# Attention on one core: row maxima from a one-pass rough score, and scores computed already turned

## The reference

```python
# attention: q, k, v of (2, 8, 576, 64), s of (2, 8, 576)
scores = q @ k.T / sqrt(64)
cum = cumsum(maximum(s, 0))
bias = -(cum[:, None] - cum[None, :])            # decay
scores = where(causal, -1e9, scores + minimum(bias, 0))
attn = exp(scores - max(scores));  attn /= sum(attn) + 1e-9
x = attn @ v                                     # 1152 tokens of 512
# then a sparse mixture of 8 experts (top 2 of noisy gate logits),
# then a dense mixture of 8 experts whose weights are balanced in 8 Sinkhorn rounds
```

## Time and profile before

| | us |
|---|---|
| median of 3 runs | 1273.04 (1272.57 to 1276.03) |
| the profiled execution's own time | 1273.47 |
| its span, first to last instruction | 1271.7 |
| TensorE busy in the span | 1220.6 (96%) |
| VectorE, ScalarE, GpSimd busy | 504.1, 373.2, 108.9 |

### The profile page before, as it was taken

The page is one execution under the profiler, slowest core; times in us unless marked ns, Lnnn a source line. Parts: engine busy times, 40 slices in busy tenths (PEclk is TensorE's granted clock), DMA queues, the critical chain, the costliest instruction groups (busy, mean ns, idle before and its releaser), DMA issues.

```text
span 1271.7 us, 17649 instructions
## 1 busy us (share of the span) xinstructions
PE 1220.6 (96%) x6721; PEld 1093.6 (86%) x6721; DVE 504.1 (40%) x1140; ACT 373.2 (29%) x678; POOL 108.9 (9%) x83
## 2 busy tenths in 40 slices
PE   5999759999999979999999999999999999999998
PEld 4989658888888868999999999999999999999997
DVE  4666665555555541443233233124214214213311
ACT  3666424444444432122122122122113113112110
POOL 2333110011110441000000000000000000000000
PEclk9999869999999979999999999999999999999999
DMA  9690405455554523011012002001101101100000
GB/s 226 179 244 12 143 26 178 178 178 178 178 178 175 164 80 133 1 66 67 1 55 78 0 7 100 25 0 66 66 0 66 66 0 66 66 0 0 25 25 25
DMA packets 23927, 105.54 MB, mean 83 GB/s; under 512 B 4400, under 2 KB 9008, under 8 KB 19792
## 3 DMA queue, kind: packets, MB, share of 16 engines
q1 hardware_dynamic: 17456, 88.51, 20.6%
q0 software_dynamic: 3360, 11.01, 3.0%
q10 hardware_dynamic: 3072, 5.51, 1.3%
HBM read 94.76 MB, written 10.26 MB: 83 GB/s over the span
## 4 chain that ended last, share of the span: by engine, by line
PE 91%; DMA 3%; DVE 3%; issue 1%; ACT 1%; SPq 1%; POOL 0%; POOLq 0%; DVEq 0%; ACTq 0%
PE bank L597 14%; PE bank L596 14%; PE bank L595 14%; PE bank L577 13%; PE bank L579 13%; PE bank L578 13%; PE bank L517 3%; DMA k_raw<-in_kT 2%; PE bank L498 2%; PE bank L480 1%; PE bank L483 1%; PE bank L541 1%; PE bank L629 1%; DMA x_sb<-x_dram,gather_at 1%; PE bank L482 0%
## 5 line engine op out<-in xcount | busy, mean ns | idle before, releaser
L577 PE MATMUL bank<-xTh,w1h 128*128 128x384 f32 (+1 forms) x1024 | 343.2, 335 | 3.0 <-DVE xTl L997 1.6
L578 PE MATMUL bank<-xTl,w1h 128*128 128x384 f32 (+1 forms) x1024 | 340.8, 333 | 0.0
L579 PE MATMUL bank<-xTh,w1l 128*128 128x384 f32 (+1 forms) x1024 | 340.7, 333 | 0.0
L792 ACT ACTIVATE hh<-bank 128x384 fp32r<-128x384 f32 (+1 forms) x256 | 123.1, 481 | 655.0 <-PE bank L579 655.0
L597 PE MATMUL bank<-w2h,hl 128*128 128x512 f32 (+1 forms) x768 | 302.3, 394 | 0.0
L596 PE MATMUL bank<-w2l,hh 128*128 128x512 f32 (+1 forms) x768 | 300.7, 392 | 0.0
L595 PE MATMUL bank<-w2h,hh 128*128 128x512 f32 (+1 forms) x768 | 299.8, 390 | 0.0
L1017 DVE SCALAR_TENSOR_TENSOR hl<-bank,hh 128x384 fp32r<-128x384 f32 (+1 forms) x256 | 139.5, 545 | 367.4 <-ACT hh L792 367.4
L577 PEld LDWEIGHTS bank<-xTh,w1h 128*128 128x128 f32 x1024 | 193.9, 189 | 5.5 <-issue 2.1
L578 PEld LDWEIGHTS bank<-xTl,w1h 128*128 128x128 f32 x1024 | 194.0, 189 | 1.2
L579 PEld LDWEIGHTS bank<-xTh,w1l 128*128 128x128 f32 x1024 | 193.8, 189 | 0.0
(11 more groups left out here) (169 smaller groups left out, 699.7 us busy)
## 6 DMA issues: line engine op xcount, KB each, us to landing
raw<-in_w SPq DMA_DIRECT2D x16, 2048.0 KB, 8.6
raw<-in_w1b SPq DMA_DIRECT2D x8, 2048.0 KB, 7.7
raw<-in_w2b SPq DMA_DIRECT2D x8, 2048.0 KB, 7.6
q_raw<-in_qT SPq DMA_DIRECT2D x16, 288.0 KB, 5.8
k_raw<-in_kT SPq DMA_DIRECT2D x16, 288.0 KB, 7.3
cumj<-cum_dram SPq DMA_DIRECT2D x8, 576.0 KB, 7.8
y_dram<-x_sb ACTq DMA_DIRECT2D x16, 256.0 KB, 4.1
x_dram<-x_sb SPq DMA_DIRECT2D x1, 2304.0 KB, 9.3
```

The lines of the kernel that those rows point to most:

```text
L577: pe.matmul(dst, w1h[:, c, fs], xTh[:, c, ts], start=(c == 0), stop=False)
L578: pe.matmul(dst, w1h[:, c, fs], xTl[:, c, ts], start=False, stop=False)
L579: mm = pe.matmul(dst, w1l[:, c, fs], xTh[:, c, ts], start=False, stop=(c == DC - 1))
L792: act.activation(hh[:, f, 0:n_cols], bank[:, f % UP_BANKS, 0:n_cols], ACT.Relu).then_inc(st.hh_ready, 1)
```

## The change

- Steps now run through one half after the other (`unit_of(k)` is `k // 5`); within a half the exact scores go through tiles of keys, not of queries.
- A new `rough` matmul, 11 steps ahead on TensorE: high part of q against high part of k, in one pass, with two more contraction rows, in which ones meet the high part and remainder of the cumulative sum. VectorE (`row_max`) adds the causal mask in SBUF and takes the negated maximum of the row into the third column of `aug`.
- TensorE turns those columns (`turn_max`, two groups a half), and ScalarE places them (`place_max`) as rows 64 to 66 of `q_top`, below the high part of q.
- `scores` computes the transposed score of one tile of keys against all later queries: `k_top` (high part of k, two rows of the cumulative sum, one of ones) against `q_top`, then `k_two` (high part over remainder) against `q_two` (remainder over high part). Decay and maximum arrive as contraction rows.
- ScalarE takes the exponential straight from PSUM into `probT`. The transposes of probabilities, their copies and the mask matmul are gone. GpSimd cuts the diagonal tile with an `affine_select` (`cut`), for which `mix` waits.
- q is loaded once and k twice; the second places of the high parts are filled by SBUF to SBUF DMAs on SP's queue (`double_k`, `double_q`). GpSimd takes the remainders in eight pieces of 288 columns a head, between its cuts.
- `k_top` lies in the memory of `w1l`, `k_two` in `w2h`, `q_top` in `w2l`; GpSimd's remainder of `w1` therefore waits for the last exact score.
- At the start three more small VectorE operations split the cumulative sum into two parts, and two rows of it are stored and reloaded.

```diff
--- before
+++ after
...
+        q_top = [w2l_flat[0:AUG, i * N:(i + 1) * N] for i in range(HEADS_RING)]
+        k_top = [w1l_flat[0:AUG, i * N:(i + 1) * N] for i in range(HEADS_RING)]
+        k_two = [w2h_flat[:, i * N:(i + 1) * N] for i in range(HEADS_RING)]
...
+        MAX_BANKS, MAX_AT, SCORES_AT, OUT_AT = 3, 3, 4, 6
+        ROUGH_AHEAD, SCORES_AHEAD = 11, 3
+
+        LOW_CHUNKS = 4
+        LOW_COLS = N // LOW_CHUNKS
+        LOWS = 2 * LOW_CHUNKS
+        K_HIGH_AHEAD, Q_HIGH_AHEAD, LOW_AHEAD = 16, 15, 13
...
+        def turns_at(k):
+
+            first, rest = divmod(k + ROUGH_AHEAD - 3, STEPS), divmod(k + ROUGH_AHEAD - 6, STEPS)
+            found = []
+            if first[1] == 0 and 0 <= first[0] < G:
+                found.append((first[0], 0))
+            if rest[1] == 0 and 0 <= rest[0] < G:
+                found.append((rest[0], 1))
+            return found
+
+        TURNED = ((3, 4), (0, 1, 2))
...
         @block.sync
...
+                w = h % HEADS_RING
+                sp.dma_start(k_top[w][HD:HD + 1, :].bitcast(F32), cum_dram[h:h + 1]).then_inc(cum_loaded[w], 16)
+                sp.dma_start(k_top[w][HD + 1:HD + 2, :].bitcast(F32), low_dram[h:h + 1]).then_inc(cum_loaded[w], 16)
+
+            def double_k(h):
+                w = h % HEADS_RING
+                sp.wait_ge(k_high, h + 1)
+                sp.dma_start(k_top[w][0:HD, :].bitcast(F32), k_two[w][0:HD, :].bitcast(F32)).then_inc(k_doubled[w], 16)
+
+            def double_q(h):
+                sp.wait_ge(q_high, h + 1)
+                sp.dma_start(q_two[HD:P, h % Q_RING, :].bitcast(F32), q_top[h % HEADS_RING][0:HD, :].bitcast(F32)).then_inc(q_doubled[h % Q_RING], 16)
...
+                sp.wait_ge(low, LOWS * (h - 1))
+                load_raw(h)
+                if h >= HEADS_RING:
+                    sp.wait_ge(scores_ready, HEAD * (h - HEADS_RING + 1))
+                    load_cum(h)
                 if h >= V_RING:
-                    sp.wait_ge(mixed, HEAD * (h - V_RING + 1) + RING)
-                load_v(h)
+                    sp.wait_ge(mixed, HEAD * (h - V_RING + 1))
+                    load_v(h)
                 if h == 4:
                     for c, g in enumerate((wg, wn, gate2)):
                         sp.dma_start(gates[:, :, c * E:(c + 1) * E], g).then_inc(gates_loaded, 16)
                     sp.dma_start(raw1[:], w1[0]).then_inc(SP_.raw1_loaded, 16)
                     sp.dma_start(raw2[:], w2[0]).then_inc(SP_.raw2_loaded, 16)
-
-            sp.wait_ge(head_done, G + 4)
+                double_k(h)
+                sp.wait_ge(scores_ready, HEAD * (h - Q_RING + 1))
+                double_q(h)
...
         @block.gpsimd
...
+            def low_part(h, c, k):
+                cols = slice(c % LOW_CHUNKS * LOW_COLS, (c % LOW_CHUNKS + 1) * LOW_COLS)
+                if c < LOW_CHUNKS:
+                    if c == 0:
+                        if h and k <= 0:
+                            pool.wait_ge(low, LOWS * h)
+                        pool.wait_ge(q_high, h + 1)
+                        if h >= Q_RING:
+                            pool.wait_ge(scores_ready, HEAD * (h - Q_RING + 1))
+                    to, raw, high = q_two[0:HD, h % Q_RING, cols], q_raw[:, h % RAW_RING, cols], q_top[h % HEADS_RING][0:HD, cols]
+                else:
+                    if c == LOW_CHUNKS:
+                        pool.wait_ge(k_high, h + 1)
+                    pool.wait_ge(low, LOWS * h + c)
+                    if k > 0:
+                        pool.wait_ge(causal_done, k)
+                    to = high = k_two[h % HEADS_RING][HD:P, cols]
+                    raw = k_raw[HD:P, h % RAW_RING, cols]
+                pool.tensor_tensor(to, raw, high.bitcast(F32), ALU.subtract).then_inc(low, 1)
+
+            def cut(k):
+                h, c = low_at(k)
+                if h is not None and c >= LOW_CHUNKS:
+                    pool.wait_ge(low, LOWS * h + c + 1)
+                n, j = unit_of(k), k % STEPS
+                wide = rows_in(j)
+                pool.wait_ge(prob_ready, k + 1)
+                diag = probT[0:wide, n % UNIT_RING, PROB_AT[j]:PROB_AT[j] + wide]
+                pool.affine_select(out=diag, in_=diag, pattern=[[1, wide]], compare_op=ALU.is_ge,
+                                   fill=0.0, base=0, channel_multiplier=-1).then_inc(causal_done, 1)
+
+            for k in range(-LOW_AHEAD, ALL):
+                h, c = low_at(k)
+                if h is not None:
+                    low_part(h, c, k)
+                if k >= 0:
+                    cut(k)
...
+            pool.wait_ge(scores_ready, ALL)
             for c in range(DC):
...
         @block.tensor
...
+            def rough(k):
+                h, b, t = head_of(k), half_of(k), rough_tile(k)
+                w, rows, width = h % HEADS_RING, rows_in(t), min(S, (t + 1) * P)
                 if k % HEAD == 0:
+                    pe.wait_ge(q_high, h + 1)
+                    if h == 0:
+                        pe.wait_ge(k_first, 1)
+                    else:
+                        pe.wait_ge(k_doubled[w], 16 * (h // HEADS_RING + (w > 0)))
+                    pe.wait_ge(cum_loaded[w], 32 * (h // HEADS_RING) + 32)
+                if k >= 2:
+                    pe.wait_ge(max_ready, k - 1)
+                first = (0, 2, 0, 1, 2)[k % STEPS]
+                q = q_top[w][0:HD + 2, b * S + t * P:b * S + t * P + rows]
                 for c0 in range(0, width, BANK):
                     c1 = min(width, c0 + BANK)
+                    mm = pe.matmul(bank[0:rows, first + c0 // BANK, 0:c1 - c0], q, k_top[w][0:HD + 2, b * S + c0:b * S + c1],
+                                   start=True, stop=True)
+                mm.then_inc(rough_ready, 1)
+
+            def turn_max(n, part):
+                tiles = TURNED[part]
+                pe.wait_ge(max_ready, STEPS * n + (2 if part == 0 else STEPS))
+                if n or part:
+                    pe.wait_ge(max_placed, 2 * n + part)
+                for t in tiles:
+                    rows = rows_in(t)
+                    at = (t - tiles[0]) * P
+                    mm = pe.transpose(bank[0:3, MAX_AT, at:at + rows], aug[0:rows, n % MAX_RING, t, :], ident[0:rows, 0:rows])
+                mm.then_inc(max_turned, 1)
+
+            def scores(k):
+                n, h, b, s_ = unit_of(k), head_of(k), half_of(k), k % STEPS
+                w = h % HEADS_RING
+                if k % HEAD == 0:
+                    pe.wait_ge(low, LOWS * (h + 1))
+                    pe.wait_ge(q_doubled[h % Q_RING], 16 * (h // Q_RING) + 16)
+                if s_ == 0:
+                    pe.wait_ge(max_placed, 2 * n + 2)
+                if k >= 2:
+                    pe.wait_ge(prob_ready, k - 1)
+                pieces = ((s_, s_ * P, S if s_ else ST * P, 0),) if s_ < ST else ((0, ST * P, S, 0), (ST, ST * P, S, HALF))
+                for j, i0, i1, at in pieces:
+                    wide = rows_in(j)
+                    c = slice(b * S + j * P, b * S + j * P + wide)
+                    r_ = slice(b * S + i0, b * S + i1)
+                    dst = bank[0:wide, SCORES_AT + k % 2, at:at + i1 - i0]
+                    pe.matmul(dst, k_top[w][:, c], q_top[w][:, r_], start=True, stop=False)
+                    mm = pe.matmul(dst, k_two[w][:, c], q_two[:, h % Q_RING, r_], start=False, stop=True)
                 mm.then_inc(scores_ready, 1)
...
-            def turn(k):
...
+            for k in range(-ROUGH_AHEAD, ALL):
+                if k + ROUGH_AHEAD < ALL:
+                    rough(k + ROUGH_AHEAD)
+                for n, part in turns_at(k):
+                    turn_max(n, part)
+                if 0 <= k + SCORES_AHEAD < ALL:
                     scores(k + SCORES_AHEAD)
-                if k + TURN_AHEAD < ALL:
-                    turn(k + TURN_AHEAD)
-                mix(k)
+                if k >= 0:
+                    mix(k)
...
         @block.scalar
...
             def exponentials(k):
+                n, s_ = unit_of(k), k % STEPS
+                act.wait_ge(scores_ready, k + 1)
+                if s_ == 0 and n >= UNIT_RING:
+                    act.wait_ge(mixed, STEPS * (n - UNIT_RING + 1))
+                src = bank[:, SCORES_AT + k % 2, :]
+                to = probT[:, n % UNIT_RING, :]
+                if s_ < ST:
+                    at, cols = PROB_AT[s_], S - s_ * P if s_ else ST * P
+                    act.activation(to[:, at:at + cols], src[:, 0:cols], ACT.Exp, scale=1.0 / SQRT_D).then_inc(prob_ready, 1)
+                else:
+                    act.activation(to[:, ST * P:S], src[:, 0:HALF], ACT.Exp, scale=1.0 / SQRT_D)
+                    act.activation(to[0:HALF, PROB_AT[ST]:PROBS], src[0:HALF, HALF:P], ACT.Exp, scale=1.0 / SQRT_D).then_inc(prob_ready, 1)
+
+            def place_max(n, part):
+                tiles = TURNED[part]
+                b, w = n % B, n // B % HEADS_RING
+                i0 = tiles[0] * P
```

(21 more changed lines are left out.)

370 lines of the change are left out of this document (146 added, 224 removed).

## The result

Four executions of the changed kernel took 1348.92 to 1351.92 us, median 1350.76; four of the kernel before, run beside them, 1273.39. The ratio is 1.060 (95% interval 1.058 to 1.062). The change makes the kernel 6% slower, 77 us, where I forecast 1274.3 and a range of 1262 to 1286.

What follows compares the result with a forecast made beforehand. TensorE was taken to bound attention (91% of the chain of waits). Terms -7.2 - 2.6 + 8.7 + 2.9 - 0.5 gave +1.3 on the median 1273.04: 1274.3 us, range 1262 to 1286.

Steps and rivals of the forecast that it cites:

- The start: Start of attention: rough scores at 11.5 us, first mix at 21, half clock until about 26; 2.6 us less lost.
- Rival C: Attention: more hand-overs keep the clock at half longer at the start and after the stall, costing 5.5 us: 1280; chance 0.12.
- A head of TensorE: Attention: TensorE's work per head falls from 14.66 to 13.76 us; eight heads save 7.2 us.
- exact score pairs: TensorE's exact scores, per half head: pairs without the mask, priced at 2.37 us at full clock.
- the maxima: TensorE's turns of five maxima per half head: priced at 0.45 us, bounds 0.15 to 0.66.
- The stall at head 4: TensorE at head 4's first rough score waits for k's copy behind the weights: 8.7 us, lower bound 5.
- The clock behind it: After head 4's stall the clock falls to half for 5.8 us, costing 2.9 us (1.5 to 3.5).
- GpSimd: Attention: low part and cut take 1.2 us an iteration; mixes wait only above 1.44; zero cost, bounds 0 to 15 us.
- Rival B: Attention: GpSimd bounds the mixes at 1.6 us an iteration, 10 us more in eight heads: 1284; chance 0.20.
- "Nothing" for the later remainders of w1: After attention: w1's low parts end about 9 us after it instead of 1.4, at no cost.
- The end: Between last mix and token turns: one finish instead of two, 1.2 instead of 1.7 us, 0.5 saved.
- rival A: Head 4 does not stall, the copy landing in time or weights draining faster: 1262.7; chance 0.30 together with a partial stall.

Runs made afterwards that it cites:

- x3: Changed kernel with rough and exact scores' first products over 128 rows, exponentials of a thousandth of the score; 1300.05 us.
- y4: Changed kernel with rough and exact scores over 128 rows, and the gates and 2 MB weight loads moved behind heads 3, 4 and 6's copies; 1317.08 us.
- v4: Changed kernel, rough and exact scores over 128 rows, weights in 512 KB quarters behind v of heads 3 to 6, no burst; median 1272.72 us, ratio 0.9981.
- x2: Changed kernel with each exact score's first product over 128 rows, the added rows zero; 1328.42 us.
- f1: Changed kernel, weight quarters behind v, burst of 12 ahead of exact score 0, GpSimd's w1 remainders held until VectorE split the gate weights; 1264.79 us, ratio 0.992.
- x1: Changed kernel with 40 extra full-height 512-column products ahead of exact score 20; 1358.32 us.
- y3: Changed kernel, exact scores' first product over 128 rows, gates and 2 MB weight loads moved behind heads 3, 4 and 6's copies; 1354.60 us.
- z2: Changed kernel, exact scores' first product over 128 rows, weight quarters behind heads 3 to 6's copies, burst of 16; 1273.38 to 1277.80 us (eight), 1315.31 to 1315.70 (three).
- x4: Kernel before with each score's first product over 64 rows instead of 128, q's remainder times k's high part left out; 1401.94 us.
- v3: Kernel before with each score's first product over 64 rows, and 40 extra full-height products ahead of score 20; 1410.32 us.
- y2: Changed kernel, gates and 2 MB weight loads moved behind heads 3, 4 and 6's copies, 40 full-height products ahead of exact score 20; 1321.60 us.
- z1: Changed kernel, weights in 512 KB quarters behind heads 3 to 6's copies, burst of 16 ahead of exact score 0; 1274.91 us once, 1312.91 to 1318.41 three times.

## Why the prediction was wrong, point by point

- **The step that failed is the clock.** The start was priced with the clock "at half clock until about 26", then full; every later term uses full-clock distances. That took the rise as a given of the stage, though it was a property of before's stream. What the runs showed in its place: attention stays at 1.2 GHz to its end, which costs 73.0 us by the first token turn. What kept the clock down are the 66 and 67 rows of the two score products: with 128 rows in both, and the same distances between products, it rises by itself (x3, y4, v4). Rival C named the mechanism ("the clock is at half for longer") and priced it at 5.5 us, chance 0.12. Its argument against, that from 150 to 155 us TensorE is busy 3.14 of 5 us and the clock is full, counts busy time alone. Those products are 128 rows high; in attention of after TensorE is busy 20.00 of 20.00 us, and the clock is at half. The Trainium skill (TensorE: Matmul & The Clock Gate, "What's actually happening") ties the clock to how busy the engine has been; by that alone attention would have run at 2.4 GHz. The trace does not agree, and the measurement decides.
- **A head of TensorE: right.** 13.4 to 13.5 us where the clock was full (x2, f1), against 13.76 predicted and 14.66 before; at half clock 24.6 (halves of 12.1 to 12.4). Eight at 24.6 instead of 14.66 are 79.5 us more, and the shorter last head gives some of it back: that is the loss. In f1 the exact score pairs take 2.03 us of a half, from start to start (0.57 for the one at 76.10, priced 0.60), against 2.37 priced; the maxima 0.35 at 75.75 and 0.25 at 80.62, 0.60 a half against 0.45, inside its bounds. That is twice the estimate of 0.3 us that stands beside that term, so three-column loads did not make the turns that cheap.
- **The start: near.** First TensorE work at 12.10 us (predicted 11.5), first exact score at 19.33 (17.3), first mix at 24.14 (21).
- **The stall at head 4: right where it could be seen.** 9.6 us in x1 and 6.4 in x2 (forecast 8.7, lower bound 5), ended by the copy behind the weights (in x1 issued at 86.72 us, landed 15.4 us later). In after it is absent, because at half pace TensorE gets there later. **The clock behind it, priced at 2.9 us, is the second step that failed:** in x1 and x2 it never came back before the end of attention, in x3 after 58 us. x2 is the case of the forecast, with the clock up at 26.8 us and the stall there, and it takes 1328.42 us beside 1274.05.
- **GpSimd: right.** A quarter of a low part takes 0.79 us (predicted 0.66 to 0.78), the cut 0.29 (priced at 0.28); at full clock GpSimd is busy 62.4 of 106.2 us and TensorE does not wait for it (f1). Rival B falls.
- **"Nothing" for the later remainders of w1: wrong.** I looked only at who needs w1, not at who runs beside GpSimd. In after a cast takes 2.02 us and a small two-operand operation 2.21, and the next token turns wait 2.24 us; at full clock the wait is 5.96.
- **The end:** one finish, 1.37 us of waiting (predicted 1.2). The 1.7 us that I gave for before is the wait of its weight loads; that of its matmuls is 1.56.

So rival A's time was there to be had: with the load order, the start and the GpSimd wait put right, f1 measures 1264.79, near A's 1262.7, with twelve extra products whose results are overwritten. The nearness is partly luck: A's terms are 10.3 us, all of them ahead of the token turns, and f1 is 7.75 us ahead of before there; its burst costs some of it, and what it gains behind that point no term of mine foresaw. Nor would the clock's rise alone have saved the forecast: x2 has the rise and misses by 54 us, because the stall takes the clock away for good.

What stays open: why rows that add nothing to the result matter to the clock; whether y3 against x2 is chance or the chip, with one execution each; why x3's clock came back and y4's did not; whether z2's falls come from the 1.9 us wait; why a 64-row product beside 128-row ones stretches the distances in x4 and v3, and whether that or the rows kept x4's clock down.

## What to carry to other kernels

Before taking products off TensorE, ask what the clock will do with what is left: count how many of the remaining products use all 128 contraction rows (in after the mixes and one of each exact pair still did, and it wasn't enough), price every later step at both levels, and carry the half-clock sum as a case with a real chance when tall products are traded for shorter ones. Unrecorded clock is not full clock: check a duration of one known shape at the stage's start and in its middle. If a kernel ends up near the edge, keep loads that stall it off the queue ahead of small copies, bring the clock up at the start with full-height work, and only then judge the arithmetic.

## What the runs showed of the hardware

- TensorE, busy without a break for some 180 us, stayed at 1.2 GHz with the changed kernel's 66- and 67-row products. Over 128 rows in both kinds of score, with the same distances from start to start, the clock rose by itself near 25 us in x3, y4 and all ten executions of v4; with the exact scores alone over 128 rows, the added ones zero, it rose in x2 and not in y3.
- Reaching and holding the 2.4 GHz level are different: the stream of y2 stayed at half for 44 us of solid work, and held full for 57.3 us once a burst of forty 512-column products over 128 rows had brought it up.
- The cost of a stall is not its length: behind idle stretches of 6.36 us (x2) and 2.22 us (y2) the clock stayed at half to the end of attention, 117 and 50 us later. In z1 it fell 0.9 us after a wait of 1.28 us; its long executions are some 40 us above its short one (1312.91 to 1318.41 against 1274.91), though only a long one was traced.
- A product over 64 rows followed by one over 128 is dearer than two over 128: 0.85 against 0.54 us for the 512-column pair at full clock (v3, before).
- VectorE's cast and two-operand operations of 0.16 to 0.23 us took 1.99 to 2.25 while GpSimd ran its subtractions of 2.46 us (9.84 us for four), and each ended as one of those did: these end at 132.94, 135.40 and 137.86 us by even parts of the row, the three operations at 132.91, 135.39 and 137.89. By the Trainium skill (SBUF — State Buffer, "SBUF: two separate sides") the two engines share a port pair that one holds for its whole instruction; f1, which adds one wait and so changes the order alone, agrees: 0.16 to 0.23 us again.
